# TensorE's loop over three batches of an attention and first-layer stage, written out

## What is computed

```python
for t in range(S):
    cur = np.einsum('bhd,bhe->bhde', u[None] * kt, vt)
    y[:, :, t] = np.einsum('bhd,bhde->bhe', rt, state + cur)
    state = w[None, :, :, None] * state + np.einsum('bhd,bhe->bhde', kt, vt)
```

```python
h = np.maximum(np.maximum(x @ w1, x @ w2), x @ w3)
x = h @ w_out
# per token: the two best of x @ w_gate + log1p(exp(x @ w_noise)) * noise, with softmax weights
out[mask] += top2_w[mask, k, None] * (np.maximum(x[mask] @ w1[e], 0.0) @ w2[e])
```

## Time and profile before

| | |
|---|---|
| median of 3 runs | 881.33 us (880.65 to 881.97) |
| the profiled execution | 881.67 us |
| its span, first to last instruction | 879.6 us |
| TensorE busy | 866.0 us, 98% of the span |
| VectorE, ScalarE, GpSimd busy | 51%, 31%, 44% |
| granted TensorE clock | 0.997 of full speed |

### The profile page before, as it was taken

How to read it: one execution, slowest core, us unless ns; L and a number is a source line. 1 busy time by engine, 2 the same in 40 slices (tenths; PEclk the granted TensorE clock), 3 DMA queues, 4 the chain that set the end, 5 groups by cost and what they waited for, 6 DMA issues and landing times. The chain is left out here.

```text
span 879.6 us, 19598 instructions
## 1 busy us (share of the span) xinstructions
PE 866.0 (98%) x6562; PEld 847.0 (96%) x6563; DVE 450.6 (51%) x1100; ACT 270.9 (31%) x520; POOL 388.0 (44%) x380
## 2 busy tenths in 40 slices
PE   7999999999999999999999999999999999999997
PEld 5999999999999999999999999999999999999997
DVE  7674646546464655636574564352525335264322
ACT  4441323223141322225414342431414233143211
POOL 5254335334352534325444555453534425365543
PEclk9999999999999999999999999999999999999999
DMA  9795112222221221032215622624326262442222
GB/s 227 176 302 134 44 45 64 65 59 54 61 57 49 67 54 38 1 122 69 46 47 191 186 67 55 185 61 138 122 57 195 70 189 75 125 150 61 72 63 68
DMA packets 103765, 86.08 MB, mean 98 GB/s; under 512 B 60634, under 2 KB 93090, under 8 KB 103696
## 3 DMA queue, kind: packets, MB, share of 16 engines
q1 hardware_dynamic: 82704, 31.56, 15.2%
q0 software_dynamic: 12416, 26.28, 9.8%
q10 hardware_dynamic: 8576, 27.33, 9.6%
HBM read 70.46 MB, written 21.35 MB: 104 GB/s over the span
## 5 line engine op out<-in xcount | busy, mean ns | idle before, releaser
L1415 PE MATMUL ps<-yh,wh 128*128 128x384 f32 x432 | 148.3, 343 | 1.7 <-ACT x_sb L1198 0.6
L1306 ACT ACTIVATE gh<-ps 128x384 fp32r<-128x384 f32 x136 | 66.9, 492 | 264.6 <-PE ps L1417 264.6
L1417 PE MATMUL ps<-yh,wl 128*128 128x384 f32 x432 | 145.1, 336 | 0.0
L1415 PE MATMUL ps<-xgh,w1h 128*128 128x384 f32 (+1 forms) x456 | 145.0, 318 | 0.0
L1416 PE MATMUL ps<-yl,wh 128*128 128x384 f32 x432 | 145.0, 336 | 0.0
L1417 PE MATMUL ps<-xgh,w1l 128*128 128x384 f32 (+1 forms) x456 | 145.0, 318 | 0.0
L1416 PE MATMUL ps<-xgl,w1h 128*128 128x384 f32 (+1 forms) x456 | 144.9, 318 | 0.0
L1062 DVE SCALAR_TENSOR_TENSOR gl<-ps,gh 128x384 fp32r<-128x384 f32 x136 | 75.8, 557 | 126.8 <-ACT gh L1306 126.8
L1415 PE MATMUL ps<-w2h,gh 128*128 128x384 f32 x408 | 138.3, 339 | 0.8 <-DVE gl L1056 0.8
L1416 PE MATMUL ps<-w2l,gh 128*128 128x384 f32 x408 | 136.5, 335 | 0.0
L1417 PE MATMUL ps<-w2h,gl 128*128 128x384 f32 x408 | 136.5, 335 | 0.0
(11 more groups left out here) (202 smaller groups left out, 1514.0 us busy)
## 6 DMA issues: line engine op xcount, KB each, us to landing
ew_raw<-ew ACTq DMA_DIRECT2D x28, 768.0 KB, 4.7
v_sb<-vN SPq DMA_DIRECT2D x24, 192.0 KB, 3.0
out<-zrow SPq DMA_DIRECT2D x1, 4608.0 KB, 16.0
x_rows<-x_sb ACTq DMA_DIRECT2D x8, 576.0 KB, 3.9
kn_sb<-kN SPq DMA_DIRECT2D x20, 192.0 KB, 2.9
k_raw<-kT SPq DMA_DIRECT2D x48, 72.0 KB, 2.5
wraw<-moe_w SPq DMA_DIRECT2D x6, 576.0 KB, 7.0
e_raw<-ew SPq DMA_DIRECT2D x4, 768.0 KB, 5.1
```

What stands on the lines that cost most here:

```text
L1306: act.activation(gh[:, f, :], ps[f % 4][:, 0:T], ACT.Relu).then_inc(gh_ok, 1)
L1415: pe.matmul(o, ah, bh, start=start, stop=False)
L1417: return pe.matmul(o, al, bh, start=False, stop=stop)
```

## The change

TensorE's loop over batches 1 to 3 becomes a loop of the program that writes the kernel, so its six periods stand one behind the other in TensorE's instructions. All numbers in them are constants. Nothing else is changed, and the other four engines' instructions are the same in both.

```diff
             fold(1, range(3))
             pe.wait_ge(fold_ok, 1)
             period(0, 0, 1, True, False, first=True)
-            with pe.Fori(1, BATCH) as b:
+            for b in range(1, BATCH):
                 for half in range(2):
                     period(2 * b - 1 + half, b, half, True, True)
             period(NBLK - 1, None, 0, False, True, final=True)
```

## The result

The changed kernel is slower: 883.95 us, median of 22 runs (881.71 to 887.03), against 881.77 of the kernel before, median of 22 runs (880.28 to 883.2). The ratio is 1.0025, with a 95% interval of 1.0018 to 1.0032, so 2.2 us. The profiled execution took 884.96 us, its span 882.9.

A forecast was written before the change was run, and what follows sets the result against it. TensorE was taken as the bound; of 1.63 us lost at its two jumps back, 0.56 + 0.26 = 0.82 us would return, VectorE keeping the rest, so 881.33 becomes 880.5 us, range 879.2 to 881.9.

The forecast's parts named there:

- What bounds the kernel: Whole kernel: TensorE is the bound, busy for 866.0 of 879.6 us, so only what delays it counts.
- what a jump back costs: TensorE's two jumps back in the first layer: 0.92 and 0.71 us with the cold start, in all 1.63 us.
- Register instructions: TensorE's loop: removing them returns 0, since the sequencer's lead of 3 us covers them.
- more fetches in straight-line code: TensorE's written-out periods: as many instructions fetched as before, code without a loop runs at the loop's pace, taken as 0.
- Rival C: Periods 1 to 6: straight-line fetches stall TensorE at block boundaries, six stalls cost 4.9 us, kernel 885.4 us; chance 0.03.
- What is late next: At both jumps TensorE waits for VectorE's first maximum, late after its own jump; gains 0.56 and 0.26, sum 0.82 us.
- The moved code: Code behind TensorE's loop: added instructions move it; 0 in the sum, any cost left to the rivals.
- rival D: Loop over experts: its moved code begins to miss, three jumps back lose 2.1 us each, kernel 886.8 us; chance 0.04.
- More instructions to fetch: TensorE's longer program: as many instructions executed and fetched as before, taken as 0, the other end left to the rivals.
- The prediction's own sign of being wrong: Anywhere outside the two jump places: the forecast is wrong if anything moves by more than 0.2 us.
- The price of a stall: TensorE's waits: each costs its idle time plus 0.11 us for the cold start of the next matmul.

The follow-up runs named there:

- after_shift32_dve: Changed kernel with 32 semaphore increments nothing waits for in period 7, and VectorE's loop written out: 887.02 us, ratio 0.9990 to the kernel before.
- after_mid16_dve: Changed kernel with 16 semaphore increments nothing waits for in each of periods 1 to 6, and VectorE's loop written out: 886.01 us, ratio 0.9977 to the kernel before.
- after: The changed kernel as first measured, TensorE's loop written out against the kernel before: 883.95 us, ratio 1.0025.
- after_again: The changed kernel as it is, run again in a later group: 888.71 us, ratio 1.0016 to the kernel before on the same chip.
- before_shift152: Kernel before, loop kept, with 152 semaphore increments nothing waits for from period 7 on: 892.61 us, ratio 1.0054 to the kernel before.
- before_again: The kernel before, unchanged, run again for its trace on the chip of a later group: 887.99 us, one run.

## Why the prediction was wrong

- **What bounds the kernel, and what a jump back costs: right.** Both stalls vanished, and the next period starts at 0.18 us.
- **Register instructions and more fetches in straight-line code at nothing: right.** The six periods run at the old pace. Rival C did not occur. The fetches are not as many as before, as I had said, but five fewer: 37 on queue q8, where there were 42.
- **What is late next: right in kind.** TensorE waits for VectorE's first maximum exactly there, at 0.05 to 0.06 us from release to matmul and 0.11 to 0.12 for the cold start. The first place gave 0.55 us, forecast 0.56. The second gave 0.50, forecast 0.26, because VectorE was idle for 3.39 us and not 3.65. The sum of the gain, forecast 0.82, was 1.04 in the shown pair. That VectorE's jump keeps the rest was tested from both sides: with it written out periods 1 to 6 lost another 0.6 and 0.9 us (after_shift32_dve, after_mid16_dve), and alone it gained nothing. VectorE's branch itself took at most 0.07 us; the idle time of 3.5 us stands behind it.
- **The moved code, at nothing in the sum, and rival D, "where it lies should not matter by so much": this step failed.** Under "More instructions to fetch" I took 0 and left the other end to the rivals. I had given D 0.04, looked only at jumps back, whose targets are still held, and dismissed the place of the code. What decided is a forward jump taken for the first time, over 282 instructions, more than a block. Its stall was 2.53 us, from one jump and not three, and by that alone the gain was turned into a loss of 1.5. The prediction's own sign of being wrong, anything outside the two places that moves by more than 0.2 us, came here.
- **The price of a stall: a term was missing.** I priced a stall with its idle time and a cold start of 0.1 us. After 2.4 and 2.6 us of idleness the clock fell in both profiled executions (after and after_again), for another 1.64 and 1.65 us of time; how often it does so in the others is the estimate given above. The 0.6 to 0.8 us idle at the jumps back had not done this in the profiled execution.

Not settled is what decides in which executions the clock falls, and how much of the median's 2.2 us is due to it. In before_shift152 TensorE stood for 2.32 us in the profiled execution and its clock stayed up behind it. Nor was the kernel tried with less code between that branch and its target, which by this account would take the sensitivity away.

## What to carry to other kernels

Code that is written out or added moves everything behind it, and a forward jump over more than a block of instructions, or one that lands just ahead of a boundary, can then stall where none did: TensorE stood for 0.4 to 2.6 us here. After such an edit look at the longest duration of each branch in the trace, and not only at the place of the edit. Removing the jump back of the bounding engine's loop paid here only as far as VectorE's own jump, at the same moment, let it.

## What was not expected of the hardware

- A fast branch of 376 ns with a stall of 1.64 us behind it: the landing place's distance to the next block boundary counts too, and not only the jump itself.
- The Trainium skill ("Runtime: NRT & Kernel Launch", "Instruction fetch mechanics") says that only two blocks are held. Here the loop over experts, from about instruction 4,610 to 5,857 before, ran its later passes with branches of at most 0.22 us, and the trace has no fetch on queue q8 from 522 us to the end. So TensorE holds at least the five blocks that it touches.
- The kernel before took 888 us on two of the chips and 882 on the third. TensorE's time in period 0 was 55.7 us on one of them (before_again), and 52.0 in the shown trace; another 1.9 us were lost in the two early tiles. Why is open. The comparisons are within one chip for that reason.
